# Last two heads of a clustered attention reordered, and two pieces of the expert routing's features turned within the last head but one

## What is computed

```python
q_assign = np.argmax(np.einsum('bhsd,hcd->bhsc', q_n, c_n), axis=-1)
k_assign = np.argmax(np.einsum('bhsd,hcd->bhsc', k_n, c_n), axis=-1)
mask = q_assign[:, :, :, None] == k_assign[:, :, None, :]
scores = scale * np.matmul(q, k.transpose(0, 1, 3, 2))
scores = np.where(mask, scores, -1000000000.0)
scores = scores - np.max(scores, axis=-1, keepdims=True)
attn = np.exp(scores)
attn = attn / (np.sum(attn, axis=-1, keepdims=True) + 1e-09)
attn_out = np.matmul(attn, v)
# x: heads side by side, 1536 x 512; then, in each of two layers,
logits = xc @ w_gate
e_idx = np.argmax(logits, axis=1)
h = np.maximum(xc[mask] @ w1[e], 0.0)
y[mask] = gate_w[mask, None] * (h @ w2[e])
```

## Time and profile before

| | |
|---|---|
| Median of 3 runs | 687.02 us (686.66 to 688.13) |
| The profiled execution's own time | 687.14 us |
| Its span in the trace | 685.4 us |
| TensorE busy | 659.6 us (96%) |
| VectorE busy | 408.1 us (60%) |
| ScalarE busy | 337.4 us (49%) |
| GpSimd busy | 294.1 us (43%) |
| Attention block | to about 268.3 us |
| Step 14 on TensorE | about 235.6 to 249.5 us |

### The profile page before, as it was taken

One profiled execution on the slowest core, in us unless ns is written; L12 is line 12 of the kernel. 1 busy time (PEld: TensorE's weight loads), 2 busy tenths in 40 slices (PEclk: granted clock), 3 DMA queues, 4 the chain that ended last, 5 costly groups with the idle time before them and its releaser, 6 DMA issues.

```text
span 685.4 us, 15560 instructions
## 1 busy us (share of the span) xinstructions
PE 659.6 (96%) x5942; PEld 565.2 (82%) x5952; DVE 408.1 (60%) x850; ACT 337.4 (49%) x506; POOL 294.1 (43%) x286
## 2 busy tenths in 40 slices
PE   8989999999999988999999999879999999999995
PEld 5569888888888876489989998548998999999894
DVE  7878888788888857755456635374335245443421
ACT  5568999999999886240343321331213214231200
POOL 4358999989999871022222312011221132122121
PEclk9999999999999999999999999999999999999998
DMA  9301221111221439758499962844456555941001
GB/s 283 91 2 47 59 82 49 47 48 48 60 82 26 128 143 330 284 152 291 174 332 369 346 223 105 294 167 149 156 173 203 214 171 184 368 172 46 20 31 32
DMA packets 45998, 105.91 MB, mean 155 GB/s; under 512 B 5459, under 2 KB 11603, under 8 KB 45936
## 3 DMA queue, kind: packets, MB, share of 16 engines
q1 hardware_dynamic: 38464, 87.65, 37.3%
q0 software_dynamic: 4544, 12.70, 5.8%
q10 hardware_dynamic: 2928, 4.72, 2.0%
HBM read 87.64 MB, written 13.11 MB: 147 GB/s over the span
## 4 chain that ended last, share of the span: by engine, by line
PE 54%; DVE 3%; DMA 2%; issue 1%; ACT 0%; POOL 0%; POOLq 0%; ACTq 0%; DVEq 0%
PE hT_ps_layer L1386 27%; PE y_ps_layer L1399 7%; PE y_ps_layer L1403 7%; PE y_ps_layer L1406 7%; PE x_turn_layer L1372 2%; PE hT_ps_layer L1327 1%; DMA x<-x_mid 1%; PE hT_ps_layer L1314 1%; PE hT_ps_layer L1312 1%; PE x_turn_layer L1302 1%; DVE row_one_hot_layer L1204 1%; DMA x_mid<-y_out_layer,y_token_layer 0%; PE count_ps_layer L1302 0%; DVE tile_gate_parts_layer L1235 0%; PE rank_ps_layer L1302 0%
## 5 line engine op out<-in xcount | busy, mean ns | idle before, releaser
L1386 PEld LDWEIGHTS hT_ps_layer<-xT_layer,w 128*128 128x128 f32 x1664 | 189.7, 192 | 2.5 <-DVE xT_layer L1247 0.4
L1386 PE MATMUL hT_ps_layer<-xT_layer,w 128*128 128x128 f32 x1664 | 189.9, 275 | 0.0
L440 POOL TENSOR_TENSOR probs_lo<-probs,probs_hi 128x768 f16<-128x768 f32 x89 | 146.3, 1652 | 33.3 <-ACT probs_hi L355 31.1
L1134 ACT ACTIVATE hT_hi_layer<-hT_ps_layer 128x512 fp32r<-128x512 f32 x52 | 31.1, 598 | 239.9 <-PE hT_ps_layer L1386 239.9
L567 DVE TENSOR_REDUCE max_halves<-turn 128x1 f32<-128x384 f32 x180 | 94.7, 553 | 32.0 <-PE turn L731 30.4
L347 ACT ACTIVATE probs<-scores 128x768 f32<-128x768 f32 x96 | 80.0, 833 | 11.3 <-PE scores L759 10.3
L1274 DVE SCALAR_TENSOR_TENSOR hT_lo_layer<-hT_ps_layer,hT_hi_layer 128x512 fp32r<-128x512 f32 x52 | 34.6, 689 | 84.3 <-ACT hT_hi_layer L1134 71.5
L1450 POOL DMA_INDIRECT out_dram<-y_out_layer,y_token_layer x16 | 19.8, 1237 | 149.7 <-DVE y_out_layer L1285 149.7
L355 ACT ACTIVATE probs_hi<-scores 128x768 f16<-128x768 f32 x96 | 80.3, 836 | 1.2 <-PE pv L783 0.9
L1254 DVE TENSOR_TENSOR w_lo<-w,w_hi 128x1024 fp32r<-128x1024 f32 x64 | 74.0, 1220 | 0.0
L1129 ACT ACTIVATE w_hi<-w 128x1024 fp32r<-128x1024 f32 x64 | 62.5, 1048 | 18.8 <-issue 18.8
(11 more groups left out here) (221 smaller groups left out, 1086.3 us busy)
## 6 DMA issues: line engine op xcount, KB each, us to landing
w<-in_moe_w_dram SPq DMA_DIRECT2D x32, 2048.0 KB, 9.5
w<-in_v_dram ACTq DMA_DIRECT2D x4, 768.0 KB, 7.1
qk_raw<-in_q_dram SPq DMA_DIRECT2D x16, 192.0 KB, 3.2
qk_raw<-in_k_dram SPq DMA_DIRECT2D x16, 192.0 KB, 3.4
qB<-qA SPq DMA_DIRECT2D x16, 192.0 KB, 2.7
kB<-kA SPq DMA_DIRECT2D x16, 192.0 KB, 3.2
x_src<-x SPq DMA_DIRECT2D x2, 1536.0 KB, 17.1
x_mid<-x SPq DMA_DIRECT2D x2, 1536.0 KB, 18.4
```

Of the source, the lines that this page charges most:

```text
L440: nc.gpsimd.tensor_tensor(p_lo[slot][:], probs[slot][:], p_hi[slot][:], ALU.subtract).then_inc(p_lo_pool, 1)
L1386: t = nc.tensor.matmul(hp[n][:, i * P:(i + 1) * P], W1[par][:, c, f * P:(f + 1) * P], xT[:, c, :], start=(c == 0), stop=(c == CD - 1))
```

## The change

With `LAST` = 15:

- **Values a step sooner.** ScalarE's `split_v(15)` and `scale_v(15)` move from step 15 to the end of step 14. In step 15 `exp_high(14, 5)` now comes before `evac_m(15)`.
- **Last scores sooner.** `scores(15, 5)` moves from the beginning of step 16 to step 15, between `weigh_hi(15, 1)` and `weigh_hi(15, 2)`.
- **VectorE adds up two heads.** `add_up` of heads 14 and 15 goes from GpSimd to VectorE; the order of `rest`, `out` and `add_up` on VectorE in steps 15 and 16 is written anew.
- **Two pieces turned in step 14.** Pieces 0 and 1 of the first layer's routing need only heads 0 to 3 and 8 to 11. TensorE turns them (`turn_chunk`) in step 14 into `lgp`, the bank of the cluster logits, which is not in use then. VectorE makes both parts (`chunk`), the first between the reductions u = 3 and 4, the second between u = 9 and 10. The first layer's routing starts with piece 2 (`EARLY` = 2). The buffers for the parts are held throughout the program.
- `WARM_MAXIMUM` is 6, not 4.

```diff
-    ... WARM_MAXIMUM = 16, 5, 3, 4, 3, 3, 3, 4, 4
+    ... WARM_MAXIMUM = 16, 5, 3, 4, 3, 3, 3, 4, 6
...
 # ScalarE, step(s)
                     exp_full(s - 1, 5)
-                    evac_m(s)
-                    split_v(s)
-                    exp_high(s - 1, 5)
+                    if s < LAST:
+                        evac_m(s)
+                        split_v(s)
+                        exp_high(s - 1, 5)
+                    else:
+                        exp_high(s - 1, 5)
+                        if s == LAST:
+                            evac_m(s)
                     exps(s, 0)
-                scale_v(s)
+                if s < LAST:
+                    scale_v(s)
...
                 evac_b(s + 2)
+                if s == LAST - 1:
+                    split_v(LAST)
+                    scale_v(LAST)
...
 # GpSimd
             def add_up(h):
-                if not live(h):
+                if not live(h) or h >= LAST - 1:
                     return
...
 # VectorE
+            def add_up(h):
+                if live(h):
+                    dve.wait_ge(out_steps, OUT_STEPS * h + OUT_STEPS)
+                    nc.vector.tensor_tensor(X(h), o_attn[:], o_mean[:], ALU.add).then_inc(x_done, 1)
+
+            def chunk(c):
+                dve.wait_ge(chunk_turned, c + 1)
+                nc.vector.tensor_copy(ahead.x_hi(c), lgp[:]).then_inc(chunk_hi, 1)
+                dve.wait_ge(chunk_hi, c + 1)
+                nc.vector.tensor_tensor(ahead.x_lo(c), lgp[:], ahead.x_hi(c).bitcast(F32), ALU.subtract).then_inc(chunk_lo, 1)
...
+                if s == LAST - 1:
+                    maximum(LAST, *range(4))
+                    chunk(0)
+                    maximum(LAST, 4, 5, 6)
+                    out(s - 1)
+                    maximum(LAST, 7, 8, 9)
+                    chunk(1)
+                    maximum(LAST, 10, 11)
+                    return
+                if s == LAST:
+                    rest(s - 1, 5)
+                    out(s - 1)
+                    rest(s, 0, 1)
+                    add_up(s - 1)
+                    rest(s, 2, 3, 4)
+                    return
+                if s > LAST:
+                    rest(s - 1, 5)
+                    out(s - 1)
+                    add_up(s - 1)
+                    return
                 maximum(s + 1, *range(7))
-                rest(s - 1, 5)
-                rest(s, 0)
                 out(s - 1)
                 maximum(s + 1, 7, 8)
                 masks(s + 2)
-                rest(s, 1, 2, 3, 4)
...
 # TensorE
+            def turn_chunk(c):
+                pe.wait_ge(x_done, LAST - 2)
+                pe.wait_ge(max_steps, MAX_STEPS * LAST)
+                if c > 0:
+                    pe.wait_ge(chunk_lo, c)
+                for i in range(ahead.GROUP):
+                    ins = nc.tensor.transpose(lgp[:, i * P:(i + 1) * P], ahead.x_part(i, c), ident[:])
+                ins.then_inc(chunk_turned, 1)
...
-                    scores(s - 1, 5)
+                    if s <= LAST:
+                        scores(s - 1, 5)
...
                     scores(s, 0)
+                    if s == LAST - 1:
+                        turn_chunk(0)
                     maxima(s + 1, 4)
...
                 maxima(s + 1, 7, 8)
+                if s == LAST - 1:
+                    turn_chunk(1)
                 assign(s + 2, 1)
...
                 weigh_hi(s, 1)
+                if s == LAST:
+                    scores(s, 5)
                 weigh_hi(s, 2)
...
 # routing, ScalarE, VectorE and TensorE; EARLY = 2 in the first layer, 0 in the second
             for k in range(NG * CD):
-                act.wait_ge(r_turned, k + 1)
-                if k >= TURNS:
-                    act.wait_ge(r_logits, k - TURNS + 1)
-                nc.scalar.activation(xh[k % TURNS][:], tr[k % TURNS][:], ACT.Copy).then_inc(r_hi, 1)
+                if k >= EARLY:
+                    act.wait_ge(r_turned, k - EARLY + 1)
+                    if k >= TURNS:
+                        act.wait_ge(r_logits, k - TURNS + 1)
+                    nc.scalar.activation(xh[k % TURNS][:], tr[k % TURNS][:], ACT.Copy).then_inc(r_hi, 1)
...
-            for k in range(NG * CD):
-                dve.wait_ge(r_hi, k + 1)
+            for k in range(EARLY, NG * CD):
+                dve.wait_ge(r_hi, k - EARLY + 1)
...
-            for k in range(TURNS - 1):
+            for k in range(EARLY, TURNS - 1):
                 route_turn(k)
```

More of the change, by code:

```diff
@@ L157, in attention @@
     p_lo_dve = sem("p_lo_dve")
+    chunk_turned = sem("chunk_turned")
+    chunk_hi = sem("chunk_hi")
+    chunk_lo = sem("chunk_lo")
     pv_hi_done = sem("pv_hi_done")
@@ L206, in bank_free @@
             pe.wait_ge(masks_in, 2 * masks_before[kind, h, n] + 2)
+    LAST = HEADS - 1
     def rest_by_dve(h, kt):
@@ L215, in attention @@
             rest_count[h, kt] = 1 + sum(rest_by_dve(*o) == rest_by_dve(h, kt) for o in rest_count)
-    WARM_START, WARM_CEN, WARM_ASSIGN, WARM_SECOND, WARM_MASKS, WARM_MAX, WARM_SCORES, WARM_TURNED, WARM_MAXIMUM = 16, 5, 3, 4, 3, 3, 3, 4, 4
+    WARM_START, WARM_CEN, WARM_ASSIGN, WARM_SECOND, WARM_MASKS, WARM_MAX, WARM_SCORES, WARM_TURNED, WARM_MAXIMUM = 16, 5, 3, 4, 3, 3, 3, 4, 6
     def wait(eng, s, value):
@@ L942, in copy_batch, with experts @@
     eng.dma_start(rows, Xt[:, :, b, :]).then_inc(copied, 16)
-def experts(nc, new, layer, Xt, consts, wg, W, wsems, dram, weights_next):
+def experts(nc, new, layer, Xt, consts, wg, W, wsems, dram, weights_next, x_parts):
     sb, ps, sem = ((lambda *a, make=make: make(f"{a[0]}_layer{layer + 1}", *a[1:])) for make in new)
@@ L951, in experts @@
     source, result, x_copy, copied, src_copied, x_loaded = dram
+    xh, xl = x_parts
     W1, W2, W2H, W2L = W
@@ L960, in experts @@
     gate_at = 1 if first else 0
+    EARLY = 2 if first else 0
     X = Xt[:].rearrange("p t b r -> p (t b) r")
-    TURNS = 4
+    TURNS = len(xh)
     NG, GT = NM // 4, 4
@@ L966, in experts @@
     wgs = sb("gate_weights_hi_lo", [P, CD, 2 * G], F32R)
-    xh = [sb(f"xT_hi{i}", [P, GT * P], F32R) for i in range(TURNS)]
-    xl = [sb(f"xT_lo{i}", [P, GT * P], F32R) for i in range(TURNS)]
     lgT = [sb(f"gate_logits_T{i}", [2 * G, GT * P], F32) for i in range(2)]
@@ L1298, in route_turn @@
                     pe.wait_ge(x_loaded[g], 32)
-                if k >= TURNS:
-                    pe.wait_ge(r_lo, k - TURNS + 1)
+                if k >= TURNS + EARLY:
+                    pe.wait_ge(r_lo, k - TURNS - EARLY + 1)
                 for i in range(GT):
@@ L1310, in route_logits @@
                     pe.wait_ge(r_copied, g - 1)
-                pe.wait_ge(r_hi, k + 1)
+                if k >= EARLY:
+                    pe.wait_ge(r_hi, k - EARLY + 1)
                 nc.tensor.matmul(logitT_ps[g % 2], wgs[:, c, :], xh[k % TURNS][:], start=(c == 0), stop=False)
-                pe.wait_ge(r_lo, k + 1)
+                if k >= EARLY:
+                    pe.wait_ge(r_lo, k - EARLY + 1)
                 nc.tensor.matmul(logitT_ps[g % 2][0:G, :], wgs[:, c, 0:G], xl[k % TURNS][:], start=False,
@@ L1499, in clustered_attention_and_experts @@
         W2 = [sb(f"w2_{i}", [P, CF, DM], F32) for i in range(2)]
+        x_parts = [[sb(f"xT_{part}{i}", [P, 4 * P], F32R) for i in range(4)] for part in ("hi", "lo")]
         made = sem("made")
@@ L1524, in clustered_attention_and_experts, with x_part, x_hi, x_lo @@
             MADE = 14
+            GROUP = 4
+            @staticmethod
+            def x_part(i, c):
+                return Xt[:, i // B, i % B, c * P:(c + 1) * P]
+            @staticmethod
+            def x_hi(c):
+                return x_parts[0][c][:]
+            @staticmethod
+            def x_lo(c):
+                return x_parts[1][c][:]
             @staticmethod
@@ L1591, in clustered_attention_and_experts @@
                 experts(nc, allocators(ctx), layer, Xt, consts, wg[layer], (W1, W2, W2H, W2L), (w1_ready, w2_ready, w1_free, w2_free),
-                        (x_src if layer == 0 else x_mid, x_mid if layer == 0 else out, x_mid, copied, src_copied, x_loaded), weights_next(layer))
+                        (x_src if layer == 0 else x_mid, x_mid if layer == 0 else out, x_mid, copied, src_copied, x_loaded), weights_next(layer), x_parts)
 _INS = ['q', 'k', 'v', 'centroids', 'moe_w_skip', 'moe_w_gate', 'moe_w1', 'moe_w2', 'moe2_w_gate', 'moe2_w_output_gate', 'moe2_w1', 'moe2_w2']
```

## The result

The changed kernel takes 688.59 us (median of 13 executions, 686.50 to 691.43) against 686.66 (13, 685.90 to 688.77) for the kernel before on the same chip: ratio 1.0032, 95% interval 1.0016 to 1.0047. It is slower by 0.3%, outside the range. The profiled execution took 690.73 us, span 689.0, mean granted clock 0.990 (before: 687.14, 685.4 and 0.994). So a part of its 3.6 us goes with the clock, and I read every stretch against a landmark near it. For the last heads that is `turn_m(14)`.

A forecast was written before the change was run, and what follows sets the result against it. It took hand-offs between four engines to bound the last heads and TensorE alone the routing's turning. Boundary +0.7 and routing -0.9 gave -0.2 us on the median of 687.02: 686.8, range 685.4 to 688.2.

The forecast's parts named there:

- The rest: Remaining parts: two more filling matmuls before a 0.73 us wait, and SyncE's big loads starting earlier; both forecast to change nothing.
- something slower that I don't see: Unnamed slower outcome, at no stated place and of no stated size; chance 0.03.
- The price of the pieces in step 14: VectorE needs 1.37 us a piece; the first makes TensorE's `u` = 9, and all of step 15, 1.36 us late.
- Values sooner: ScalarE, steps 14 to 15: scaling values a step sooner shrinks the 1.36 us delay to 0.60 at `exp_full(15, 1)`.
- Last scores sooner: Step 15: TensorE waits at `scores(15, 5)`, so `weigh_lo(15, 5)` starts 0.69 us late; the old order would be 0.2 late.
- rival B: Step 15: the new place of `scores(15, 5)` holds nothing up, ScalarE sets the end; total -0.7, 686.3 us; chance 0.13.
- VectorE adds up two heads: Attention's end: sums take 0.56 us each on VectorE, TensorE's drain stays last; gain 0 to 0.1 us.
- Two pieces less in the routing: First layer's routing: TensorE saves the transposes of two pieces, 0.9 us, bounds 0.88 to 1.06.
- rival C: First layer's routing gains nothing, ScalarE or VectorE taking over as its bound; +0.7, 687.7 us; chance 0.06.
- Rival D: Step 14: GpSimd shuts out VectorE's four piece instructions, 0.8 us each, together +2.05; 688.9 us; chance 0.07.
- Rival A: Step 14 hides the turning in idle time, step 15 starts 1.36 us sooner; total -1.6, 685.4 us; chance 0.11.

The follow-up runs named there:

- before_pad8: Kernel before plus eight already-met waits on VectorE at the start of the second layer's routing; 688.19 us against 686.84, ratio 1.0018.
- after_l2pad4: Changed kernel plus four already-met waits on VectorE at the start of the second layer's routing; 687.52 us against 687.14 for the kernel before, ratio 1.0004.
- late_early4: Changed kernel with both pieces moved behind VectorE's `out(13)`, plus four already-met waits near VectorE's first instructions; 686.73 us against 686.84 before, ratio 0.9989.
- after_early4: Changed kernel plus four already-met waits near VectorE's first instructions; 687.64 us against 686.84 for the kernel before, ratio 1.0006.
- scores_old_place: Changed kernel with the last scores back at the beginning of step 16; 687.13 us against 687.49 for the kernel before, ratio 0.9996.
- late_l2pad4: Changed kernel with both pieces behind `out(13)`, plus four already-met waits on VectorE at the second layer's routing; 685.72 us against 687.14 before, ratio 0.9981.
- after_third: The changed kernel itself measured a third time, for its clock; 688.52 us against 686.84 for the kernel before, ratio 1.0017.
- before_pad4: Kernel before plus four already-met waits on VectorE at the start of the second layer's routing; 686.87 us against 687.49, ratio 0.9991.
- no_turn: Changed kernel without the two pieces in step 14, the routing turning all 12; 686.99 us against 687.10 for the kernel before, ratio 0.9999.
- turn_only: Kernel before with only the two pieces turned in step 14 and the shorter routing, buffers held throughout; 688.31 us against 687.10, ratio 1.0019.
- after_pad124: Changed kernel plus 124 already-met waits on VectorE at the second layer's routing; 690.40 us against 687.49 for the kernel before, ratio 1.0045.

## Why the prediction was wrong

**The step that failed is the last one of the sum, "The rest": it had no term for VectorE's code outside the attention.** I went through what the change does to queues, buffers and clocks and priced what I saw. That four instructions more on one engine move the places where its chains stop was in neither the sum nor a rival; "something slower that I don't see" had 0.03. The runs showed for it +0.67 us in the second layer (reproduced by `before_pad8` without the change, all but gone in `after_l2pad4`), and 0.36 inside `out(13)`: in each kernel with `chunk(0)` ahead of it, and in `late_early4`, where two waits have its place (in `after_early4`, with both, it is one operation further on and about 0.2). This step alone doesn't carry the time out of the range, as the sum below shows; that takes the clock's part, whose cause stays open.

**The price of the pieces in step 14: right mechanism, size off.** From a piece's start to the next instruction it is 1.33 us (1.37 forecast); `u` = 9 late by 1.69 (1.36). The difference is the stop in `out(13)`, 0.46 for 0.10; without it 1.33, my walk to 0.03. `turn_m(15)` is +1.69.

**Values sooner: right, a little less.** The order and every duration came as walked, and the delay shrank by 0.70 us, from 1.69 to 0.99, where I had 0.76, from 1.36 to 0.60. `exp_full(15, 0)` waited 0.77 us for the second half of its scores, where I had 0.71.

**Last scores sooner: right direction, wrong size.** `weigh_lo(15, 0)` 24.45 us after the landmark (24.02 by my walk), and the last products +1.13 (0.69). The wait of TensorE that I had ahead of `scores(15, 5)` isn't there: its row, 263.03, has none, and it starts 0.4 us later after the landmark than forecast. And I had put the old place at 0.5 us better; `scores_old_place` shows 0.22: the old order gives back less of the delay than I had walked (+0.91 instead of +0.2 from a start that was itself 0.39 later). So rival B's saving by that place was 0.2 us and not 0.5, and its 686.3 was out of reach.

**VectorE adds up two heads: right.** The sums take 0.55 and 0.56 us and TensorE's drain stays last. `rest(14, 5)` lasts 1.23 us for the 0.95 that it has in `late_l2pad4`, beside GpSimd's subtraction of the values; after:

```profile
256.12 1.61 POOL L461 TENSOR_TENSOR v_lo<-w,v_hi_and_one 128x384 f16<-128x384 f32 x1
```

(0.89 us is the median of the 16 heads' in the kernel before, where this one took 1.22). The two stretch each other, and it stays hidden. The Trainium skill, "SBUF — State Buffer", section "Who interferes with whom", says that a VectorE instruction with two SBUF inputs and a GpSimd one that reads SBUF exclude each other. The trace agrees: 1.23 us for 0.95 and 1.61 for 0.89.

**Two pieces less in the routing: right.** -0.96 for -0.9, so rival C is false. **Rival D** is false: the pieces took 0.69 us an instruction with GpSimd's remainders beside them. **Rival A** is false for this change, but not for its idea: behind `out(13)` both pieces are hidden (-1.52 at the last logits, forecast of A -1.6).

With what was measured the sum is 1.13 - 0.96 + 0.67 = +0.84 us; the three sets of the changed kernel give +0.94, +1.14 and +0.63 at equal clock. That would be 687.9, inside the range of 685.4 to 688.2.

**What stays open is the rest, about 0.8 us of clock.** The mean granted clock is 0.9937 over 31 executions of the changed kernel and 0.9952 over 118 of the kernel before, worth 0.0015 x 0.53 / 0.001 = 0.8 us (with the 0.84 it makes 1.6 of the 1.9 us between the first medians); the median clocks are 0.994 and 0.995. At or below 0.992 are 11 of 31 against 14 of 118 (in `after_third`, run for this question, 5 of 12). That speaks for the change causing it, but the bound of 0.992 was chosen with the numbers in sight, and other kernels with the stop at the gates show it in 5 of 43. `scores_old_place` had none in 12, which is most of why its median looks 1.4 us better than the changed kernel's. The place near 20 us has a wait for a transfer just before the clock falls, in the changed kernel's profile:

```profile
19.49 0.73 PE L863 MATMUL scores<-kB,qB 96*128 96x384 f32 x2 [0.83 <-DMA kB<-kA]
```

The start of every kernel differs from execution to execution by a microsecond or more: `before_pad4`, the same code as before up to the second layer, reached `turn_m(14)` 2.1 us later than it, with a granted clock of 0.79 from 44 to 52 us; and `no_turn`, without the pieces, had 0.66 from 18 to 28 us. Whether the change makes such falls more frequent no run here settles.

## What to carry to other kernels

When a change adds instructions to an engine, budget half a microsecond (0.36 and 0.67 here) of gain or loss in its other chains of short dependent operations, and check it by adding a few waits that are long met; a change whose forecast is smaller than that can't be judged from its own stage. Put added work on the engine behind the hand-off that others wait for, not into the largest idle sum of the step: with piece 0 ahead of `out(13)` the last products came 1.7 us later (`turn_only`: 1.3 its work, 0.4 the stop), with both pieces behind it no later. Compare kernels at equal granted clock when the difference is a few tenths of a per cent.

## What the hardware showed that I had not expected

The chain of 128x12 operations on VectorE at the second layer's gates, 0.17 us each, stops for 0.2 to 0.5 us at fixed operations, and whether it does goes with how many VectorE instructions stand ahead of it: counted from the kernel before, 0 us with 0 or 2 instructions more, 0.67 or 0.68 with 4 (five different kernels), 0.12 with 6 (four kernels), -0.01 with 66. The mechanism is not shown by any run here. Waits that are already met are not free: 62 instructions of them took 6.2 us, 0.10 us each (`after_pad124`). And 0.001 of mean granted clock, which is 1.37 us at 1.2 GHz, was worth 0.53 us of span, where 0.69 would be lost if TensorE set the pace throughout.
